# First layer in blocks of 128, 128, 256 and five of 512 tokens, with a visit of the recurrence in every second period from block 2 on

## What is computed

```python
def _attn_ref(q, k, v, alpha):
    for t in range(S):
        state = alpha[:, :, t, :, None] * state + np.einsum('bhd,bhe->bhde', k[:, :, t], v[:, :, t])
        y[:, :, t] = np.einsum('bhd,bhde->bhe', q[:, :, t], state)
...
def _moe_ref(x, w_in, w_out):        # 3072x384, 384x2048, 2048x384
    h = x @ w_in
    g = h * (1.0 / (1.0 + np.exp(-1.702 * h)))
    return g @ w_out
...
def _moe2_ref(x, w_in, w_out):       # the same shapes
    h = x @ w_in
    g = h - np.tanh(h)
    return g @ w_out
```

## Time and profile before

| | |
|---|---|
| median of 3 runs | 981.36 us (981.34 to 982.28) |
| the profiled execution's own time | 982.34 us |
| its span | 980.5 us |
| TensorE matmul busy | 955.3 us (97%) |
| VectorE busy | 532.2 us (54%) |
| ScalarE busy | 333.7 us (34%) |
| GpSimd busy | 279.0 us (28%) |

### The profile page before, as it was taken

How to read it: one execution, slowest core, us unless ns; L and a number is a source line. 1 busy time by engine, 2 the same in 40 slices (tenths; PEclk the granted TensorE clock), 3 DMA queues, 4 the chain that set the end, 5 groups by cost and what they waited for, 6 DMA issues and landing times.

```text
span 980.5 us, 22172 instructions
## 1 busy us (share of the span) xinstructions
PE 955.3 (97%) x9312; PEld 825.0 (84%) x9312; DVE 532.2 (54%) x1349; ACT 333.7 (34%) x683; POOL 279.0 (28%) x314
## 2 busy tenths in 40 slices
PE   3899999999999999999999999999999999999998
PEld 3799999999999988888888888888888888888886
DVE  7569997778788877775421213334334333343333
ACT  2342333332332332323234554333333333333332
POOL 2554756565664644444001542000000000000000
PEclk9999999999999999999999999999999999999999
DMA  8733242332332422420023322020010020200101
GB/s 218 196 70 87 49 97 55 95 67 55 94 75 53 113 57 62 104 45 18 17 65 114 98 87 89 1 65 1 1 65 1 1 65 1 65 1 0 33 1 33
DMA packets 136533, 59.08 MB, mean 60 GB/s; under 512 B 114288, under 2 KB 131824, under 8 KB 136432
## 3 DMA queue, kind: packets, MB, share of 16 engines
q1 hardware_dynamic: 132560, 53.98, 21.9%
q10 hardware_dynamic: 3872, 3.67, 1.2%
HBM read 43.47 MB, written 14.16 MB: 59 GB/s over the span
## 4 chain that ended last, share of the span: by engine, by line
PE 94%; DVE 3%; DMA 1%; issue 1%; ACT 0%; SPq 0%; DVEq 0%; ACTq 0%
PE pX L735 38%; PE pZ L759 26%; PE pX L759 14%; PE pX L614 3%; PE pX L730 2%; PE pZ L641 2%; PE pZ L694 2%; PE pZ L650 2%; PE pZ L600 2%; PE pX L627 1%; PE pZ L685 1%; DVE scores L1046 1%; DVE w_lo L1052 1%; DMA x_raw<-attn_out 0%; DMA r<-q_t 0%
## 5 line engine op out<-in xcount | busy, mean ns | idle before, releaser
L735 PE MATMUL pX<-x_hi,w_hi 128*128 128x512 f32 (+2 forms) x624 | 227.7, 365 | 0.7 <-ACT g L891 0.7
L735 PE MATMUL pX<-x_lo,w_hi 128*128 128x512 f32 (+2 forms) x624 | 227.3, 364 | 0.0
L735 PE MATMUL pX<-x_hi,w_lo 128*128 128x512 f32 (+2 forms) x624 | 227.3, 364 | 0.0
L1062 DVE TENSOR_TENSOR g_lo<-g,g_hi 128x512 fp32r<-128x512 f32 (+2 forms) x208 | 135.2, 650 | 160.2 <-ACT g_hi L896 160.1
L1161 DVE TENSOR_TENSOR g<-pX,sg 128x512 f32<-128x512 f32 x96 | 66.4, 691 | 177.6 <-ACT sg L893 177.6
L759 PE MATMUL pZ<-g_hi,w_hi 128*128 128x512 f32 (+2 forms) x414 | 151.0, 365 | 0.0
L759 PE MATMUL pZ<-g_lo,w_hi 128*128 128x512 f32 (+2 forms) x414 | 150.8, 364 | 0.0
L759 PE MATMUL pZ<-g_hi,w_lo 128*128 128x512 f32 (+2 forms) x414 | 150.8, 364 | 0.0
L896 ACT ACTIVATE g_hi<-g 128x512 fp32r<-128x512 f32 (+2 forms) x208 | 121.3, 583 | 78.1 <-DVE g L1161 74.5
L891 ACT ACTIVATE g<-pX 128x512 f32<-128x512 f32 (+3 forms) x144 | 65.6, 456 | 217.2 <-PE pX L735 179.5
L735 PEld LDWEIGHTS pX<-x_hi,w_hi 128*128 128x128 f32 x624 | 117.5, 188 | 17.9 <-ACT g L891 1.1
(11 more groups left out here) (91 smaller groups left out, 1122.9 us busy)
## 6 DMA issues: line engine op xcount, KB each, us to landing
v<-v_l SPq DMA_DIRECT2D x96, 48.0 KB, 2.4
x_raw<-hidden SPq DMA_DIRECT2D x6, 768.0 KB, 5.7
attn_out<-y SPq DMA_DIRECT2D x94, 48.0 KB, 1.9
out_t<-o SPq DMA_DIRECT2D x10, 384.0 KB, 3.5
alpha<-a_t SPq DMA_DIRECT2D x24, 128.0 KB, 3.0
r<-q_t SPq DMA_DIRECT2D x24, 128.0 KB, 3.1
k<-k_t SPq DMA_DIRECT2D x24, 128.0 KB, 3.0
w_raw<-w_in SPq DMA_DIRECT2D x16, 192.0 KB, 2.4
```

The costliest lines, as they stand in the source:

```text
L735: last = nc.tensor.matmul(pH(N)[:, 0:w], win(wp, f, m), XS[T % 2][xp][:, m, 0:w], start=(n == 0), stop=(n == len(terms) - 1))
L1062: nc.vector.tensor_tensor(GL[:, columns(N)], g_raw(N), GH[:, columns(N)].bitcast(F32), ALU.subtract).then_inc(gl_done, 1)
```

## The change

The two blocks of 384 and one of 256 are gone, and two of 512 stand in their place; layer 1 has 128 periods and not 144. The visits come at every fourth period up to N = 28 and at every second one from N = 32 on. `x_high` and `x_low` of the next block stand at period 14 of a block and not at 10 or 12; for block 1 it stays 13.

```diff
-WIDTHS = [128, 128, 256, 256, 384, 384, 512, 512, 512]
+WIDTHS = [128, 128, 256, 512, 512, 512, 512, 512]
...
-    starts = ([0, 4, 8, 12, 16, 20, 25, 30] + [33 + 3 * n for n in range(5)] + [49 + 3 * n for n in range(5)]
-              + [64 + 2 * n for n in range(29)])
+    starts = [4 * n for n in range(8)] + [32 + 2 * n for n in range(39)]
...
-X_AT = {1: 13, 3: 12}
+X_AT = {0: 10, 1: 13}
...
-            return 6 if T >= L1B - 1 else X_AT.get(T, 10)
+            return 6 if T >= L1B - 1 else X_AT.get(T, 14)
```

## The result

The changed kernel takes 1004.39 us (1004.24 to 1005.18, 4 runs) against 981.82 us of the kernel before (981.34 to 982.86, 4 runs): a ratio of 1.0231 [1.0217, 1.0246], 22.6 us slower. The profiled execution's own time is 1005.18 us, its span 1003.4, which is 22.9 above the span before.

What follows compares the result with a forecast made beforehand. TensorE bounds the kernel on average, VectorE within a hair from 78 to 108 us. Terms -3.8 + 5.8 + 2.4 + 5.4 + 6.9 + 2.4 = +19.1 us; forecast 1000 us, range 993 to 1006.

Steps and rivals of the forecast that it cites:

- the likeliest case of 997 to 1002: Whole kernel: all terms as summed, forecast 1000 us; chance 0.5.
- the rival in which the clock falls at both long waits: TensorE at N = 32 and 48: clock falls fully behind both waits, 2.4 us more, 1003; chance 0.15.
- Fewer matmuls, -3.8: TensorE, layer 1: 576 matmuls in place of 864 for the same columns, 3.8 us less, counted in full.
- Item 9 ahead of `x_lo` of block 2, +5.8: Start of block 2: TensorE waits for `x_lo`, which VectorE now does after item 9; 5.8 us lost.
- Block 2's denser visits, +2.4: Block 2, eight visits in place of five: VectorE falls behind, item 17's scores start late; 2.4 us lost.
- The alpha wait that I spread as 0.5 a visit: VectorE in block 2: waits 0.5 us for alpha in each odd visit, 1.5 us in all.
- the rival in which GpSimd's ring becomes the bound: Block 2: alpha, queries, next alpha take 13 to 16 us a unit against 14.8; up to 1005; chance 0.13.
- `x_lo` of block 3, +5.4: N = 48: TensorE, ready at 166.8, waits for `x_lo` behind item 17's visit; 5.4 us lost.
- Three blocks more, +6.9: Block starts N = 64, 80 and 96: `x_lo` behind an odd item's visit, 2.3 us each, 6.9 us lost.
- The clock, +2.4: TensorE behind the two long waits: a possible fall to half pace, 2.4 us as middle of 0 and 4.8.
- The bound of 2.4 for one fall: TensorE behind a long wait: one clock fall costs at most 2.4 us, half of 4.8.

Runs made afterwards that it cites:

- e12_w_even: The kernel of e10_w_later with layer 1's `w_lo` spread more evenly over the periods: 983.15 us, ratio 0.9993 to the kernel before.
- e3_xfirst: Changed kernel with `x_lo` of block 2 put ahead of item 9's scores again in VectorE's program: 1001.14 us, ratio 1.0185 to the kernel before.
- e6_wlo_act: Changed kernel with layer 1's `w_lo` written by ScalarE as plain weight copies, not by VectorE (values differ): 995.05 us, ratio 1.0137 to the kernel before.
- e5_alpha2: Changed kernel with two buffers of alpha in turn, so alpha is loaded one unit earlier: 1004.26 us, ratio 1.0226 to the kernel before.
- e7_x46: Changed kernel with `x_lo` of block 3 directly behind item 17's states, ahead of its decay products: 1000.43 us, ratio 1.018 to the kernel before.
- e2_fill: Changed kernel with 22 and 21 unused filler matmuls ahead of the first `up` of N = 32 and 48: 1000.05 us, ratio 1.0177 to the kernel before.
- e4_visits: Kernel before, its blocks and `x_at` kept, with the change's visit periods alone: 1008.94 us, ratio 1.0272 to the kernel before.
- e10_w_later: Changed kernel with visits every third period up to N = 45, `x_lo` earlier, `w_lo` made later: 983.41 us, ratio 1.0011 to the kernel before.

## Why the prediction was right, step by step

The forecast was 1000 us with 993 to 1006; 1004.4 lies in that range, but not in the likeliest case of 997 to 1002. The case that came about is the rival in which the clock falls at both long waits, 1003, to which the prediction gave 0.15. The waits themselves came where the reading of VectorE's timeline put them.

- **Fewer matmuls, -3.8.** An `up` still takes 2.04 us. That it counts in full was right in the sum and of no use: e12_w_even shows that VectorE takes it back.
- **Item 9 ahead of `x_lo` of block 2, +5.8.** Measured 5.75. e3_xfirst confirms the order as its place, e6_wlo_act the backlog as its source.
- **Block 2's denser visits, +2.4.** Measured 3.1, but most of it at one visit early in the block (2.62 at N = 38) and not gathered up at its end, so that the nearness of the two numbers is partly luck. The alpha wait that I spread as 0.5 a visit came as 2.62, 0.39, 1.15 and 0.50. e5_alpha2 shows that these aren't what costs; the rival in which GpSimd's ring becomes the bound falls with it, though its time, 1005, was the nearest of all. The ring's operations didn't lengthen: the queries of the units in block 2 took 6.73, 5.88, 5.51 and 5.11 us, those of the same four units before 7.54, 5.45, 5.82 (the row) and 5.43.
- **`x_lo` of block 3, +5.4.** Measured 5.48, with everything 5 us later than I had it (ready at 171.9, not 166.8), for the clock's two falls, the later start and the waits ahead. Where the 5.4 comes from is shown by e7_x46: 2.9 of it is what stood between item 17's states and `x_lo`.
- **Three blocks more, +6.9.** Measured 6.1, and none at N = 112, as said. The row of before gave 2.2 each; the last two had it, the first 1.81.
- **The clock, +2.4: the term that was mis-sized.** Measured 5.1. I took the middle of 0 and 4.8 for two falls, an average over cases. Both falls came (1.5 and 2.3, where 2.4 each was my bound), and a third of 1.3 behind a wait of 2.62 us, where the prediction asked after none. This is 2.7 of the 3.8 us by which the sum missed the span, and 1.1 is the later start of block 2; the waits together are 20.4 us, where 20.5 were forecast. The bound of 2.4 for one fall was no bound either: in e5_alpha2 and e7_x46, behind the same wait of 5.7 to 5.8 us, a fall cost 2.6 (first `up` to second 8.02 and 8.10 us, 5.46 without a fall). It had been read from 41.14 on, but TensorE had been at work, with idle times of 0.45 us at most, since 27.75.

The Trainium skill (TensorE: Matmul & The Clock Gate, HAM oscillation) says that idle gaps in the middle of a kernel let the clock gate fall back to half rate. The trace agrees, with 0.50 behind 5.75 and 5.48 us, and e2_fill shows what it costs.

## What to carry to other kernels

Where a side engine is as full as the bound one, put what the bound engine needs next (here an input's low part) at the head of the side engine's order, and compare both engines' time for each repeated piece of work over every stretch before making it denser: a saving on the bound engine there is given back as waits. One half of a change can need the other, as the visits needed the wide blocks; try each alone. When a wait of microseconds on TensorE is expected, price a slow stretch behind it as well as the wait (1.3 to 2.6 us each here), and use filler matmuls to tell the two apart.

## What the runs showed of the hardware beyond expectation

**The length of a wait doesn't settle whether the clock falls.** Behind 2.11 us of idle time in e2_fill it read 0.56 (134 to 137, above). In e4_visits TensorE waited longer, 2.37 us, ending at 133.81, and it stayed up:

```profile
134.00:137.00 3.00, 3.00 (x115) 2.66 (x111) 3.00 (x7) 1.61 (x5) 2.92 (x4) 1.00 0.02 3
```

Over all profiles here, past the first 50 us, the shortest wait with a fall behind it, begun within 2 us of its end, is 1.46 us (e10_w_later) and the longest without one is this of 2.37; between these it went either way, for one and the same wait too: 2.15 us at N = 80 had a fall in e5_alpha2 and none in the change (2.16). Nor does the wait settle the price: behind 5.7 to 5.8 us at N = 32 the clock was still at 0.50 over 110 to 113 in e5_alpha2 and e7_x46, and at 0.86 in the change, 1.5 us of cost against 2.6.

**The granted clock isn't always recorded in the first 50 us.** Before, it read 1.00 over 39 to 42 while matmuls ran at half pace; after, with the same pace, the same stretch reads 0.50:

```profile
39.00:42.00 3.00, 2.63 (x32) 2.12 (x35) 0.00 (x0) 1.30 (x4) 0.79 (x2) 0.50 0.21 52
```

There the durations are to be believed. When the clock first rises also differs from one execution to the next, ahead of anything that was changed: between the same two `up`s TensorE takes 19.45 us in the change (35.75 to 55.20) and 15.47 in e6_wlo_act (36.52 to 51.99), whose program is the same up to there and whose clock reads 1.00 over 39 to 42. So a difference of 4 us between two single spans can be the start alone.

**Small operations of VectorE can take four times as long beside GpSimd.** The first decay step took 0.29 us at 126.63, with GpSimd idle, and 1.15 at 142.89 (rows above), where it ends at 144.04, just behind this one:

```profile
142.84 1.06 POOL L562 TENSOR_TENSOR q<-r,f 112x512 f32<-112x512 f32 x1
```

The second step took 1.08 us at 158.37 and 173.46 and ended within 0.1 us behind the same operation of GpSimd in both. The Trainium skill (SBUF — State Buffer, SBUF: two separate sides) says that the two engines share a pair of ports as a lock, and the loser blocks for a whole instruction. The rows agree in their sizes and ends; no run here isolates it.
